# Transformer mixer on one core: low parts moved to GpSimd, an absolute value moved to VectorE, one angle product moved behind the attention loop

## The reference

```
scores = q @ k^T / 8 ; scores = cap * tanh(scores / cap)
attn = softmax(scores) ; x = attn @ v            # heads side by side: (4, 448, 768)
theta = x @ w_theta                              # 768 x 768
y = w_tok_r @ (x * cos(theta)) + w_tok_i @ (x * sin(theta))
u = x + y ; x = u + relu(u @ w_ch)
h = relu(x^T @ w_tok1) @ w_tok2 ; u = x + h^T
out = u + relu(u @ w_ch1) @ w_ch2                # 768 -> 1536 -> 768
```

## Time and profile before

| what | value |
|---|---|
| median of three runs | 877.3 us |
| the profiled execution's own time | 877.85 us |
| its span | 876.1 us |
| TensorE busy | 861.5 us, 98% |
| VectorE busy | 442.0 us, 50% |
| ScalarE busy | 319.9 us, 37% |
| GpSimd busy | 126.2 us, 14% |

### The profile page before, as it was taken

The page is one execution under the profiler, slowest core; times in us unless marked ns, Lnnn a source line. Parts: engine busy times, 40 slices in busy tenths (PEclk is TensorE's granted clock), DMA queues, the critical chain, the costliest instruction groups (busy, mean ns, idle before and its releaser), DMA issues.

```text
span 876.1 us, 12475 instructions
## 1 busy us (share of the span) xinstructions
PE 861.5 (98%) x5164; PEld 734.6 (84%) x5164; DVE 442.0 (50%) x653; ACT 319.9 (37%) x383; POOL 126.2 (14%) x83
## 2 busy tenths in 40 slices
PE   8999999998999999999999999999999999999998
PEld 6545555598999999999999988888999988889998
DVE  5899999999678877534344352212310310003002
ACT  6999999665354636212213021111100100001000
POOL 0254654222000000160000033500000000000000
PEclk9999999999999999999999999999999999999999
DMA  6646764343222223300000137100400030002001
GB/s 163 170 129 171 189 176 119 102 115 86 71 55 64 52 67 108 100 15 1 1 1 0 64 108 262 53 1 1 144 1 1 0 108 1 1 1 72 1 1 55
DMA packets 57576, 61.96 MB, mean 71 GB/s; under 512 B 22288, under 2 KB 52912, under 8 KB 57520
## 3 DMA queue, kind: packets, MB, share of 16 engines
q1 hardware_dynamic: 57296, 60.94, 24.6%
q10 hardware_dynamic: 224, 0.23, 0.1%
HBM read 47.13 MB, written 14.02 MB: 70 GB/s over the span
## 4 chain that ended last, share of the span: by engine, by line
PE 81%; DVE 12%; issue 4%; ACT 1%; DMA 1%; DVEq 0%; ACTq 0%
PE psum L1083 24%; PE psum L1085 24%; PE psum L1084 24%; PE psum L1124 4%; PE psum L1095 2%; DVE tile_sums L783 2%; PE psum L1235 1%; PE psum L1098 1%; DVE kq_hi L768 1%; PE psum L1151 1%; DVE wide_lo L945 1%; DVE kq_lo L770 1%; DVE tile_sums L790 1%; DVE sum_rows L805 1%; DVE x_t L796 1%
## 5 line engine op out<-in xcount | busy, mean ns | idle before, releaser
L1066 DVE SCALAR_TENSOR_TENSOR relu_lo<-psum,relu_hi 128x512 fp32r<-128x512 f32 (+1 forms) x48 | 30.0, 624 | 271.8 <-ACT relu_hi L752 271.8
L752 ACT ACTIVATE relu_hi<-psum 128x512 fp32r<-128x512 f32 (+1 forms) x48 | 26.2, 545 | 305.4 <-PE psum L1085 295.4
L1083 PE MATMUL psum<-wide_hi,mlp 128*128 128x512 f32 (+1 forms) x288 | 104.4, 362 | 2.0 <-DVE wide_lo L945 2.0
L1085 PE MATMUL psum<-wide_hi,mlp 128*128 128x512 f32 (+1 forms) x288 | 104.2, 362 | 0.0
L1084 PE MATMUL psum<-wide_lo,mlp 128*128 128x512 f32 (+1 forms) x288 | 104.2, 362 | 0.0
L1085 PE MATMUL psum<-relu_hi,mlp 128*128 128x512 f32 (+1 forms) x288 | 104.1, 362 | 0.0
L1083 PE MATMUL psum<-relu_hi,mlp 128*128 128x512 f32 (+1 forms) x288 | 104.1, 362 | 0.0
L1084 PE MATMUL psum<-relu_lo,mlp 128*128 128x512 f32 (+1 forms) x288 | 104.1, 362 | 0.0
L1124 PE MATMUL psum<-ring,values 128*32 128x448 f32 x768 | 81.4, 542 | 0.0
L624 ACT ACTIVATE ring<-psum,score_scale 128x1344 f32<-128x1344 f32 (+1 forms) x48 | 75.3, 1569 | 9.5 <-PE psum L1098 7.1
L627 ACT ACTIVATE ring<-ring,cap_col 128x1344 f32<-128x1344 f32 (+1 forms) x48 | 77.1, 1607 | 1.6
(11 more groups left out here) (134 smaller groups left out, 1941.1 us busy)
## 6 DMA issues: line engine op xcount, KB each, us to landing
kq_raw<-kq_t SPq DMA_DIRECT2D x47, 224.0 KB, 3.8
mlp_raw<-moe_w_ch SPq DMA_DIRECT2D x24, 384.0 KB, 6.9
values<-v SPq DMA_DIRECT2D x48, 112.0 KB, 3.4
inverse_rows<-inverse_scratch SPq DMA_DIRECT2D x12, 448.0 KB, 6.5
rows_scratch<-turned SPq DMA_DIRECT2D x112, 48.0 KB, 1.7
x_rows<-rows_scratch SPq DMA_DIRECT2D x28, 192.0 KB, 2.4
u_scratch<-x_t SPq DMA_DIRECT2D x2, 1344.0 KB, 5.6
out_t<-x_t SPq DMA_DIRECT2D x4, 672.0 KB, 3.2
```

The lines of the kernel that those rows point to most:

```text
L752: act.activation(relu_hi[c % 3][:, 0:n_tokens], psum[:, c % 2, 0:n_tokens], ACT.Relu).then_inc(relu_hi_made, 1)
L1066: dve.scalar_tensor_tensor(out=relu_lo[c % 3][:, 0:n_tokens], in0=psum[:, c % 2, 0:n_tokens], scalar=0.0, in1=relu_hi[c % 3][:, 0:n_tokens ...
L1083: pe.matmul(out, left[0], right[0], start=start, stop=False)
L1085: return pe.matmul(out, left[1], right[0], start=False, stop=stop)
```

## The change

GpSimd makes the low parts of z: `make_z_lo` is gone from VectorE, and a loop over the 28 tiles stands in GpSimd's list behind the scaling of pair 19. The scaling of pairs 20 to 23 stands within that loop, before tile 4. ScalarE's absolute value is gone; VectorE takes it in `reduce_angle` as max(-a, a), an instruction with two SBUF inputs, and both sine inputs come from `reduced`. `angle(0)` has left the attention loop: it is made behind `weigh_second(23)`, and `sum_keys(23)` follows it. The last `copy_sums` moves from before the stage into n = 1, the last `invert` from n = 2 to n = 3, `make_x_lo(2)` one tile earlier, and each `add_mixed` one tile earlier. SyncE's last `store_sums`, `load_sums` and `store_inverses` stand later among `store_rows` and `load_rows`.

```diff
@@ SyncE
             load_rows(AHEAD - 1)
-            store_sums(N_PAIRS - 1)
-            load_sums(N_SUMS - 1)
             for n in range(AHEAD, N_ANGLES):
                 store_rows(n)
+                if n == AHEAD:
+                    store_sums(N_PAIRS - 1)
                 load_rows(n)
                 if n == AHEAD + 1:
+                    load_sums(N_SUMS - 1)
+                if n == AHEAD + 2:
                     store_inverses(N_SUMS - 1)
                     spread_inverses(N_SUMS - 1)
@@ GpSimd
-            for pair in range(N_PAIRS - BATCH_OF_SUMS, N_PAIRS):
-                scale_heads(pair)
+            for n, (b, half, t) in enumerate(ANGLES):
+                if n == 4:
+                    for pair in range(N_PAIRS - BATCH_OF_SUMS, N_PAIRS):
+                        scale_heads(pair)
+                    pool.wait_ge(heads_scaled, N_PAIRS)
+                pool.wait_ge(z_hi_made, 2 * (n + 1))
+                if t < 3:
+                    pool.tensor_tensor(z_lo[half][:, t, :], cos_z[n % 4][:, :],
+                                       z_hi[half][:, t, :].bitcast(F32), ALU.subtract)
+                    pool.tensor_tensor(z_lo[half][:, 3 + t, :], sin_z[n % 4][:, :],
+                                       z_hi[half][:, 3 + t, :].bitcast(F32), ALU.subtract
+                                       ).then_inc(z_lo_made, 1)
...
+            pool.wait_ge(z_lo_made, N_ANGLES)
@@ ScalarE
                 act.wait_ge(angles_ready, n + 1)
-                act.activation(cos_z[n % 4][:, :], cos_z[n % 4][:, :], ACT.Abs).then_inc(angles_folded, 1)
-                act.wait_ge(angles_folded, n + 1)
@@ VectorE, reduce_angle
-                dve.scalar_tensor_tensor(out=cos_z[n % 4][:, :], in0=t[:, :], scalar=-TWO_PI_LO,
+                dve.scalar_tensor_tensor(out=reduced[:, :], in0=t[:, :], scalar=-TWO_PI_LO,
                                          in1=reduced[:, :], op0=ALU.mult, op1=ALU.add
                                          ).then_inc(range_steps, 1)
                 dve.wait_ge(range_steps, steps + 3)
-                dve.tensor_scalar(sin_z[n % 4][:, :], cos_z[n % 4][:, :], PI_BELOW,
+                dve.scalar_tensor_tensor(out=cos_z[n % 4][:, :], in0=reduced[:, :],
+                                         scalar=-1.0, in1=reduced[:, :],
+                                         op0=ALU.mult, op1=ALU.max)
+                dve.tensor_scalar(sin_z[n % 4][:, :], reduced[:, :], PI_BELOW,
                                   -PI_BELOW, ALU.min, ALU.max).then_inc(angles_ready, 1)
@@ VectorE, its list in the stage
-            copy_sums(N_PAIRS - 1)
             for n in range(N_ANGLES):
-                if n == 2:
+                if n == 1:
+                    copy_sums(N_PAIRS - 1)
+                if n == 3:
                     invert(N_SUMS - 1)
                 reduce_angle(n)
                 for b in range(1, BATCH):
-                    if n == STARTS[2 * b] - (1 if b == 2 else 2):
+                    if n == STARTS[2 * b] - 2:
                         make_x_lo(b)
                 if n >= 1:
                     make_z(n - 1)
-                if n >= 2 and n != STARTS[1] + 1:
-                    make_z_lo(n - 2)
                 if n + AHEAD < N_ANGLES:
                     turn_rows(n + AHEAD)
-                if n == STARTS[1]:
-                    make_z_lo(n - 1)
                 for j in range(2, len(PHASE_TILES)):
-                    for m, d in ((1, 0), (1, 1), (2, 2)):
+                    for m, d in ((0, 0), (0, 1), (1, 2)):
@@ TensorE
-                else:
-                    pe.wait_ge(mix_weights_split, 9)
-                    pe.wait_ge(x_lo_made, 1)
-                    pe.wait_ge(tanh_done, group_end(pair, 0))
-                    angle(0)
                 weigh_first(pair)
                 if pair >= 1:
                     sum_keys(pair - 1)
                 weigh_second(pair)
-            sum_keys(N_PAIRS - 1)
...
+                    mm.then_inc(theta_ready, 1)
+                    if n == 0:
+                        sum_keys(N_PAIRS - 1)
```

More of the change, by code:

```diff
@@ L303, in mixer_kernel @@
         angles_ready = sem("angles_ready")
-        angles_folded = sem("angles_folded")
         trig_done = sem("trig_done")
@@ L589, in _ @@
                 scale_heads(pair)
-            for pair in range(N_PAIRS - BATCH_OF_SUMS, N_PAIRS):
-                scale_heads(pair)
+            for n, (b, half, t) in enumerate(ANGLES):
[10 more added lines that the diff above has]
+                                       ).then_inc(z_lo_made, 1)
+                else:
+                    pool.tensor_tensor(tail_lo[0][half][:, :], tail_z[0][:, :],
+                                       tail_hi[0][half][:, :].bitcast(F32), ALU.subtract)
+                    pool.tensor_tensor(tail_lo[1][half][:, :], tail_z[1][:, :],
+                                       tail_hi[1][half][:, :].bitcast(F32), ALU.subtract
+                                       ).then_inc(z_lo_made, 1)
+            pool.wait_ge(z_lo_made, N_ANGLES)
             pool.wait_ge(tok_loaded, 32)
@@ L988, in _ @@
             make_z(N_ANGLES - 1)
-            make_z_lo(N_ANGLES - 2)
-            make_z_lo(N_ANGLES - 1)
             for d in range(3):
@@ L1157, in _ @@
                 pe.transpose(psum[:, 7, 0:P], ident[:, :], ident[:, :])
[L1158 to L1171, removed]
             pe.wait_ge(masks_made, 5 + 2 * VALUE_BUFFERS)
@@ L1186, in _, with angles @@
                 weigh_second(pair)
-            sum_keys(N_PAIRS - 1)
+            def angles(j):
+                for n in range(STARTS[j], STARTS[j + 1]):
+                    b, half, t = ANGLES[n]
+                    columns = slice(half * HALF, (half + 1) * HALF)
+                    tokens = slice(t * P, (t + 1) * P)
+                    after(pe, angles_ready, n - 3)
+                    if n == 3:
+                        pe.wait_ge(sums_copied, N_PAIRS)
+                    for k in range(D_TILES):
+                        mm = products(psum[:, THETA_BANKS[n % 4], 0:HALF],
+                                      (x_hi[:, k, tokens], x_lo[:, k, tokens]),
+                                      (theta_hi[:, k, columns], theta_lo[:, k, columns]),
+                                      k == 0, k == D_TILES - 1)
+                    mm.then_inc(theta_ready, 1)
+                    if n == 0:
+                        sum_keys(N_PAIRS - 1)
             def mix_tokens(j):
@@ L1206, in mix_tokens @@
                     mm.then_inc(mixed, 1)
+            pe.wait_ge(mix_weights_split, 9)
             for j in range(len(PHASE_TILES)):
@@ L1210, in _ @@
                     pe.wait_ge(x_lo_made, j // 2 + 1)
-                for n in range(max(STARTS[j], 1), STARTS[j + 1]):
-                    angle(n)
+                angles(j)
                 if j == 1:
```

## The result

The change made the kernel slower: 886.4 us median of 5 runs (885.8 to 887.2) against 877.3 us, ratio 1.0096 with a 95% interval from 1.0075 to 1.0117. Measured again on another chip the ratio was 1.0068 (1.0041 to 1.0094). 886.9 us had been forecast, in a range from 880 to 891. The total was near; as the experiments show, two of its terms were not, and in the kernel before the place that sets the end was not the one named.

What follows compares the result with a forecast made beforehand. The prediction took VectorE's list up to `x_lo(1)`, which TensorE awaits before `angle(8)`, as the bound; 4.0 + 2.8 - 3.8 + 6.3 - 0.5 + 0.8 = +9.6 us gave 886.9 us against the median, range 880 to 891.

Steps and rivals of the forecast that it cites:

- the restart at 211.43: TensorE's start of `angle(8)` after waiting 2.4 us for `x_lo(1)`; claimed as the place to watch, any VectorE delay counting one for one.
- the third wait for `z_lo`: Last of TensorE's three short waits for `z_lo` (1.0 us together), behind the long `x_lo` wait; claimed to stay.
- A: End of attention: with `angle(0)` moved, TensorE idles 2.7 us and loses 1.3 us to half clock; +4.0 us.
- The clock term: Behind the new idle gap at the end of attention, TensorE's clock falls to half: 1.3 us lost (bounds 0 and 1.4).
- all that is queued behind is late: After the attention gap, pair 23, `angle(0)` and `angle(1)` on TensorE were claimed to come 2.7 us late.
- E: GpSimd's scalings of pairs 16 to 19 stay in time, meet `reduce_angle(0)` and cost VectorE 2.4 instead of 2.95 us; -0.5 us.
- B: VectorE's `reduce_angle`: six new absolute-value instructions on the chain up to `x_lo(1)`, 0.47 us each; +2.8 us (1.7 to 3.5).
- C: VectorE before `x_lo(1)`: eight low-part instructions of tiles 0 to 3 go, 0.47 us each; -3.8 us.
- D: Ten low-part instructions on GpSimd, tiles 0 to 4, hold VectorE up 0.63 us each; +6.3 us (0 to 11.2).
- F: Sums' last round: `load_sums` behind row transfers lands late, so VectorE waits at n = 3; +0.8 us (0 to 2).

## Why the prediction was right, by its steps

*The chain, and its end.* Right that TensorE's idle time, with the clock behind it, is all there is to win or lose in this stage, and that VectorE's list sets it. `angle(8)` was forecast near 221 and started at 220.57; counted from `make_x_lo(0)`, that is 59.5 us in both profiles after against 51.9 and 52.8 before, +7.1, where +9.6 had been added up. Wrong that the restart at 211.43 is the point that binds in the kernel before: the third wait for `z_lo`, 14 us later, is the last, and the long one before it was absorbed in it, half clock included (x_lo(1) one tile earlier gained nothing). In the changed kernel the x_lo wait is the last indeed, and the third, of which the prediction says that it stays, is gone. Behind x_lo the half clock holds for sixteen products, 220.57 to 225.53, where it was ten, about 0.9 us more, against 0.4 us of the third wait saved: from +7.1 at `angle(8)` to +7.6 for the stage.

*A, the angle (forecast +4.0).* The gap itself was right: 3.3 and 2.8 us against 2.7. The clock term was wrong: 0 instead of 1.3. And most of the rest did not arrive: 0.9 us of the stage put in alone (within the spread of the kernel before), 1.9 taken out, of which 1.3 at `angle(8)`. What failed is the step "all that is queued behind is late": the queue was late, but the scalings of pairs 16 to 19 were not, and the later `reduce_angle(1)` no longer met them.

*E (forecast -0.5).* The same step from the other side. `reduce_angle(0)` met one scaling instead of four (line 908 at 179.60 takes 1.31 us). The second fell beside the transposes and the copy of the sums, which took no longer, and the third and fourth on tile 1. In the profile after, tile 1 starts at 181.90, not 183.5, and takes 6.16 us to 188.06 where before it took 8.2 with the sums' inversion. A and E together were 3.5 in the forecast and 1 to 2 in the runs.

*B, the absolute value (forecast +2.8).* Mis-sized: 4.0 to 4.9. The length was right (179.12 to 179.60 is 0.48). Put in alone, eight count where six were counted, because the chain of the kernel before runs on to `z_lo(7)`, and it also opened waits in later phases. Taken out of the changed kernel, six count, 2.4 us, and most of the rest is the half clock behind the last wait, which the prediction took as fixed.

*C and D, the low parts (forecast -3.8 + 6.3 = +2.5).* 1.6 alone. The price per GpSimd instruction was 0.6, as scaled from the earlier trace rows. One of the five pairs, that of tile 1, cost 0.5 us instead of 1.2, as it fell in the time in which VectorE waited for the sums. The scalings of pairs 20 to 23, taken as equal, cost somewhat more than before: with the low parts of tile 3 ahead of them, tile 5 takes 9.9 us (204.13 to 214.07), 4.9 more than its own work. Of these 1.2 are the low parts and 3.7 the scalings, which cost 3.0 in the kernel before.

*F, the sums (forecast +0.8).* The wait was 1.3 us, and taking it away gave 1.6 us of the stage, 1.05 of it at `angle(8)`.

*What no step held, and luck.* TensorE waited 1.0 us for the reduced angle of tile 3 before `angle(7)`, which no step had; the wait for the low part of tile 3 grew to 2.8 us, as forecast. Both were absorbed in the wait for x_lo. VectorE's wait for ScalarE's high part before `make_x_lo(2)` ("some 3 us") did not come: it starts at 258.29 without idle time. Singly put in, three parts add up to 0.9 + 4.9 + 1.6 = 7.4 us of the stage, but the changed kernel without the new round of the sums, which holds these three together, is at +6.0 (211.2), so that they overlap, and the sums' 1.6 make the whole 7.6. The smaller moves (`copy_sums`, `make_x_lo(2)`, `add_mixed`) were not tried singly. So the forecast 9.6 stands against 9.1 between the medians of the first chip, 6 us by the ratio on the second, and 7.6 in the stage. It was a sum in which A was too large and B too small, with a race near 520 us on top that the changed kernel won in both its profiles. The direction and the size within some microseconds were earned; that the total came within a microsecond was luck.

## What to carry to other kernels

Follow the chain to the last wait, not to the longest: a wait that is followed by a smaller one of the same releaser can be taken away without any gain. When a start is moved, ask of every collision on the way whether it moves along, for work fixed by a transfer stays where it is. And an instruction given to GpSimd is not off VectorE: here each cost VectorE 0.6 us where its own version took 0.47. Last, where a wait is followed by the half clock, price the clock with it: a wait that gets shorter can give back more than its own length, as the absolute value did.

## What the runs showed of the hardware

The granted clock did not fall behind 2.75 to 3.3 us without work on TensorE at the end of attention (six profiles: 1.00), but did behind 2.44 us before `angle(8)` and in five of six profiles behind 1.6 to 1.8 us before the first product with `wide_hi`. The length of the gap alone does not decide. What does was not tried. Before `angle(8)` alone, the first 30 products took 7.8 to 8.1 us behind waits of 3.4 to 3.6 us (three profiles), 6.7 to 6.9 behind 2.0 to 2.8 (four), and 5.3 behind 0.6 to 1.7 (five).

Which of VectorE's steps GpSimd holds up can be counted over the stages of all profiles, in the cases where a GpSimd instruction was under way when the step started and had at least 0.1 us to go. The step that reads PSUM (line 897 in the changed kernel) kept to 0.56 us in all 92, and the transposes kept their length in all 45. The step on line 908 (889 before), with one SBUF input, took 1.03 to 1.33 us instead of 0.36 in all 99. So two SBUF inputs are not needed for a collision. The prediction names these alone when it explains the collisions, though line 889 in its own, 1.19 us long, has one.

Near 520 us two instructions start at most 0.3 us apart, and their order decides between 3.4 and 4.8 to 5.0 us for VectorE, and between 1.85 and 4.8 to 5.05 us for GpSimd: the first holds the second until it is through. The Trainium skill (SBUF — State Buffer, "Who interferes with whom") has this rule, that the order of issue decides who blocks; the twelve profiles in which one of the two was first agree with it.
